# Retention and mixture of experts: fewer matmul sizes in the expert loop, one leaf above 336 rows, and the last empty scatters moved ahead

## What is computed

```
logits = x @ w_gate                      # 2304 x 8
expert = argmax(logits);  gate = softmax(logits)[expert]
h = maximum(x_of_expert @ w1[e], 0)      # 512 -> 1024
y = h @ w2[e]                            # 1024 -> 512
out[row] = gate[row] * y                 # at most 576 rows an expert are kept
```

## Time and profile before

| | us |
|---|---|
| median of 3 runs (lowest, highest) | 385.37 (383.69, 397.42) |
| the profiled execution | 389.81 |
| its span | 387.9 |
| TensorE matmul busy | 359.4 (93%) |
| VectorE, ScalarE, GpSimd busy | 218.2, 187.4, 136.1 |

### The profile page before, as it was taken

The page is one execution under the profiler, slowest core; times in us unless marked ns, Lnnn a source line. Parts: engine busy times, 40 slices in busy tenths (PEclk is TensorE's granted clock), DMA queues, the critical chain, the costliest instruction groups (busy, mean ns, idle before and its releaser), DMA issues.

```text
span 387.9 us, 10976 instructions
## 1 busy us (share of the span) xinstructions
PE 359.4 (93%) x3590; PEld 339.4 (88%) x3591; DVE 218.2 (56%) x450; ACT 187.4 (48%) x367; POOL 136.1 (35%) x131
## 2 busy tenths in 40 slices
PE   8999899999998899499979999999999999998980
PEld 4999799999875799499969999999999999998980
DVE  3136634938864585356545556656666756655740
ACT  1343433436330465256445547557657657646721
POOL 3655353533505222034404503532532432222205
PEclk9999999999995999789989999999999999999997
DMA  8889989887863599925533653664664654540001
GB/s 225 238 230 305 271 228 245 259 259 232 246 185 116 172 370 368 341 71 177 196 112 133 203 159 110 197 212 155 204 200 155 199 196 147 176 162 38 25 0 54
DMA packets 27435, 73.41 MB, mean 189 GB/s; under 512 B 7114, under 2 KB 7882, under 8 KB 27408
## 3 DMA queue, kind: packets, MB, share of 16 engines
q1 hardware_dynamic: 21008, 63.57, 51.9%
q0 software_dynamic: 6400, 9.46, 8.0%
HBM read 64.61 MB, written 19.92 MB: 218 GB/s over the span
## 4 chain that ended last, share of the span: by engine, by line
PE 86%; issue 4%; DVE 4%; DMA 3%; POOL 1%; ACT 1%; DVEq 0%; ACTq 0%; POOLq 0%; SPq 0%
PE bank L620 19%; PE bank L622 18%; PE bank L621 18%; PE bank L455 5%; PE bank L479 4%; PE bank L608 4%; PE bank L469 3%; PE bank L505 3%; PE bank L498 3%; PE bank L613 3%; PE bank L487 2%; DMA qk_raw<-in_qk 2%; PE bank L558 2%; DMA y_nat<-x_rows,slot_row 1%; POOL out L382 1%
## 5 line engine op out<-in xcount | busy, mean ns | idle before, releaser
L620 PE MATMUL bank<-m_hi,w_hi 128*128 x512 | 154.8, 302 | 3.0 <-DVE m_lo L1002 1.4
L621 PE MATMUL bank<-m_hi,w_lo 128*128 x512 | 152.9, 299 | 0.0
L622 PE MATMUL bank<-m_lo,w_hi 128*128 x512 | 152.8, 298 | 0.0
L827 DVE TENSOR_TENSOR w_lo<-w_raw,w_hi 128x512 fp32r<-128x512 f32 x128 | 88.5, 691 | 33.5 <-ACT w_hi L702 33.2
L620 PEld LDWEIGHTS bank<-m_hi,w_hi 128*128 128x128 f32 x512 | 96.3, 188 | 5.9 <-issue 5.8
L621 PEld LDWEIGHTS bank<-m_hi,w_lo 128*128 128x128 f32 x512 | 96.3, 188 | 0.0
L622 PEld LDWEIGHTS bank<-m_lo,w_hi 128*128 128x128 f32 x512 | 96.2, 188 | 0.0
L702 ACT ACTIVATE w_hi<-w_raw 128x512 fp32r<-128x512 f32 x128 | 79.9, 626 | 24.9 <-PE bank L622 24.9
L382 POOL DMA_INDIRECT out<-y_nat,slot_row x40 | 41.7, 1042 | 137.1 <-PE bank L622 88.9
L1006 DVE SCALAR_TENSOR_TENSOR m_lo<-bank,m_hi 128x384 fp32r<-128x384 f32 x64 | 35.7, 558 | 38.0 <-ACT m_hi L783 38.0
L376 POOL DMA_INDIRECT x_gat<-x_rows,slot_row x37 | 41.0, 1109 | 43.6 <-PE bank L622 22.6
(11 more groups left out here) (89 smaller groups left out, 369.6 us busy)
## 6 DMA issues: line engine op xcount, KB each, us to landing
w_raw<-in_moe_w SPq DMA_DIRECT2D x64, 512.0 KB, 3.8
qk_raw<-in_qk SPq DMA_DIRECT2D x24, 384.0 KB, 4.9
kv_raw<-in_kv SPq DMA_DIRECT2D x24, 384.0 KB, 5.9
x_rows<-x_nat SPq DMA_DIRECT2D x24, 192.0 KB, 5.2
out<-zeros SPq DMA_DIRECT2D x12, 384.0 KB, 7.7
q_dec<-in_qdecay SPq DMA_DIRECT2D x5, 192.0 KB, 6.2
out<-y_nat,slot_row POOLq DMA_INDIRECT x40, 2.8
x_gat<-x_rows,slot_row POOLq DMA_INDIRECT x37, 3.9
```

The source lines that it names most:

```text
L620: pe.matmul(dst, w_hi[:, s, i, :], hi[:, i, cols], start=(i == 0), stop=False)
L621: pe.matmul(dst, w_lo[:, s, i, :], hi[:, i, cols], start=False, stop=False)
L622: last = pe.matmul(dst, w_hi[:, s, i, :], lo[:, i, cols], start=False, stop=(i == K4 - 1))
L827: dve.tensor_tensor(w_lo[:, j % SLOTS], w_raw[j // 2][:, j % 2 * 512:j % 2 * 512 + 512].rearrange("p (k n) -> p k n", k=K4), w_hi[:, j % S ...
```

## The change

- `SIZES` is now 272, 288, 304, 320, 336. The leaves of 256 and of 384 columns are gone. Expert 7 (255 rows) runs 272 columns instead of 256; the other seven keep their size.
- All counts above 336 share one leaf, `large`, with 384 columns and a test of the count around each wide part. It stands ahead of the five small leaves in the program. None of the eight experts runs it.
- In `large` the wide product comes ahead of the narrow one.
- GpSimd issues the two wide scatters of expert 7 ahead of its three narrow ones. ScalarE counts up `b_y_scaled` of an expert without wide rows ahead of its products instead of behind them.
- `keep_warm` gets a parameter that nobody uses.

```diff
-SIZES = [256, 272, 288, 304, 320, 336, WA]
+SIZES = [272, 288, 304, 320, 336]
...
-def by_count(eng, count, body, sizes=(*SIZES, None)):
-
+def by_count(eng, count, body, large, sizes=None):
+
+    if sizes is None:
+        with eng.If(count > SIZES[-1]):
+            large()
+        with eng.Else():
+            by_count(eng, count, body, large, SIZES)
+        return
     if len(sizes) == 1:
-        body(*((WA, True) if sizes[0] is None else (sizes[0], False)))
+        body(sizes[0])
         return
     half = len(sizes) // 2
     with eng.If(count <= sizes[half - 1]):
-        by_count(eng, count, body, sizes[:half])
+        by_count(eng, count, body, large, sizes[:half])
     with eng.Else():
-        by_count(eng, count, body, sizes[half:])
+        by_count(eng, count, body, large, sizes[half:])
...
+            def wide_scatters(e):
+                for g in range(NA, NG):
+                    pool.wait_ge(b_y_scaled, NB * (e - 1) + g - NA + 1)
+                    after_chunk(e, g)
+                    scatter(e - 1, g)
+
             for e in range(E + 1):
...
+                if e == E:
+                    wide_scatters(e)
                 if e > 0:
                     for g in range(NA):
                         pool.wait_ge(y_scaled, NA * (e - 1) + g + 1 + SCALED0)
                         after_chunk(e, g)
                         scatter(e - 1, g)
-                    for g in range(NA, NG):
-                        pool.wait_ge(b_y_scaled, NB * (e - 1) + g - NA + 1)
-                        after_chunk(e, g)
-                        scatter(e - 1, g)
+                if e == E:
+                    break
+                if e > 0:
+                    wide_scatters(e)
...
-                        last = product(ring[s][:, 0:n], s, hi, lo, slice(0, n))
-                        if wide:
-                            last = product(wide_ring[s][:, 0:WB], s, hi, lo, slice(WA, CAP))
-                        last.then_inc(result_made, 1)
+                        if count is not None:
+                            with pe.If(count > WA):
+                                product(wide_ring[s][:, 0:WB], s, hi, lo, slice(WA, CAP))
+                        product(ring[s][:, 0:n], s, hi, lo, slice(0, n)).then_inc(result_made, 1)
...
+            def small(e, n):
+                pe.sem_inc(b_xs_tr, NB)
+                chunks(e, n)
+                pe.sem_inc(b_y_tr, NB)
+
+            def large(e, count):
+
+                with pe.If(count > WA):
...
+                        turn_x(wide_turn[g], NA + g).then_inc(b_xs_tr, 1)
+                with pe.Else():
                     pe.sem_inc(b_xs_tr, NB)
-                    chunks(e, n, False)
+                chunks(e, WA, count)
+                with pe.If(count > WA):
...
-                by_count(pe, count, lambda n, wide: sized(e, n, wide))
+                by_count(pe, count, lambda n: small(e, n), lambda: large(e, count))
...
                     act.sem_inc(b_xs_hi_made, NB)
+                    act.sem_inc(b_y_scaled, NB)
```

More of the change, by code:

```diff
@@ L553, in add_to_map, with keep_warm @@
                 return last
-            def keep_warm(times, unused=bank[6]):
+            def keep_warm(times, unused=bank[6], n=512):
                 for _ in range(times):
-                    pe.matmul(unused[0:C, :], zeros[:, 0:C], zeros[:, 0:512], start=True, stop=True,
+                    pe.matmul(unused[0:C, 0:n], zeros[:, 0:C], zeros[:, 0:n], start=True, stop=True,
                               skip_group_check=True)
@@ L623, in product, with chunks @@
                 return last
-            def chunks(e, n, wide):
+            def chunks(e, n, count=None):
                 with pe.Fori(0, CHUNKS // SLOTS) as it:
@@ L637, in chunks @@
                             pe.wait_ge(xs_lo_made, e * NA + NA)
-                        if s == 0 and wide:
+                        if s == 0 and count is not None:
                             pe.wait_ge(b_xs_lo_made, NB * (e + 1))
@@ L644, in chunks @@
                             pe.wait_ge(y_scaled, e * NA + SCALED0)
-                        last = product(ring[s][:, 0:n], s, hi, lo, slice(0, n))
-                        if wide:
-                            last = product(wide_ring[s][:, 0:WB], s, hi, lo, slice(WA, CAP))
-                        last.then_inc(result_made, 1)
-            def sized(e, n, wide):
-                if not wide:
-                    pe.sem_inc(b_xs_tr, NB)
-                    chunks(e, n, False)
-                    pe.sem_inc(b_y_tr, NB)
[L655 to L666, removed]
+                        if count is not None:
+                            with pe.If(count > WA):
+                                product(wide_ring[s][:, 0:WB], s, hi, lo, slice(WA, CAP))
@@ new lines, in chunks @@
+                        product(ring[s][:, 0:n], s, hi, lo, slice(0, n)).then_inc(result_made, 1)
[5 more added lines that the diff above has]
+                with pe.If(count > WA):
+                    pe.wait_ge(xs_lo_made, e * NA + 2 * NA)
+                    pe.wait_ge(y_scaled, e * NA + SCALED0)
+                    for g in range(NB):
+                        pe.wait_ge(gathered[NA + g], 16 * (e + 1))
+                        turn_x(wide_turn[g], NA + g).then_inc(b_xs_tr, 1)
+                with pe.Else():
+                    pe.sem_inc(b_xs_tr, NB)
+                chunks(e, WA, count)
+                with pe.If(count > WA):
+                    pe.wait_ge(result_copied, (e + 1) * CHUNKS + COPIED0)
+                    for g in range(NB):
+                        turn_y(wide_turn[g], NA + g, min(G, WB - g * G)).then_inc(b_y_tr, 1)
+                    pe.wait_ge(b_y_scaled, NB * (e + 1))
+                with pe.Else():
+                    pe.sem_inc(b_y_tr, NB)
@@ L805, in expert @@
                         scale_y(wide_turn[g], e + 1, NA + g, min(G, WB - g * G)).then_inc(b_y_scaled, 1)
-                else:
-                    act.sem_inc(b_y_scaled, NB)
             act.wait_ge(routed, 2)
```

## The result

The changed kernel takes 396.36 us (median of five runs, 392.47 to 397.53), beside 386.54 us (383.69 to 397.42, five runs) for the kernel before: 1.0253 times as long, interval 1.0207 to 1.0299. It is slower; the forecast was 380.0 us, range 371 to 389.5. The profiled execution took 396.61 us with a span of 394.6.

What follows compares the result with a forecast made beforehand. TensorE, busy 359.4 of 387.9 us, bounds the kernel, its loop idle mostly from two late exit branches. Terms -4.1 + 1.24 - 2.58 = -5.4 us, off the median of 385.37, gave 380.0 us, range 371 to 389.5.

Steps and rivals of the forecast that it cites:

- step 3: Entry of expert 0: the jump past the large leaf to the 272 leaf costs 0, at worst +5.4 us.
- The prediction's own sign of being wrong: An entry branch over 3 us, expert 0's first matmul at 134 us or later, or a short first exit.
- rival C: Expert 0's entry misses and both exits still do: 389.5 us, up to 395.8 with expert 1's entry; chance 0.12, upper end 0.05.
- 1. The exit of expert 0: Branch out of expert 0's leaf, over 540 instructions instead of 960: still a miss, taken as 0, at best -7.6 us.
- step 2: Branch out of expert 1's leaf, over 135 instructions instead of 550: no longer waits, -4.1 us.
- 4. Expert 7: Expert 7's matmuls: 272 columns instead of 256 cost +1.24 us, all on the path.
- 5. The tail: End of the kernel: two scatters fewer behind expert 7's first narrow one, -2.58 us.
- 6. The tests: Fourth compare ahead of the 320 and 336 leaves: at most +0.2 us in two passes, taken as 0.
- Rival D: Loop branches: the code's place changes nothing, both exits wait as they did; -1.3 us, 384.0 us; chance 0.10.

Runs made afterwards that it cites:

- e1: The changed kernel with the large leaf laid behind the five small ones, one If turned round; 382.74 us, 0.9833 of the kernel before.
- e5: The changed kernel without its leaf for more than 336 rows; 381.51 us, 0.9848 of the kernel before.
- e6: The changed kernel with a branch hint at the head of TensorE's loop for its jump to the small leaves; 384.22 us, 0.9965 of the kernel before.
- e7: The changed kernel with the large leaf behind the small ones, a second time; 382.24 us, 0.9869 of the kernel before.
- e3: The kernel before with 155 never-run matmuls between the head of the pass and the tests; 400.94 us, 1.0347 of the kernel before.
- e9: The kernel of small leaves alone (e5) with its five leaves reversed, 336 first and 272 last; 390.86 us, 0.9997 of the kernel before.
- e8: The changed kernel again, without an edit; median 392.99 us of six runs, its profiled execution 382.39 us.
- e2: The kernel before with only the change's scatters and count-up, TensorE's program untouched; 398.55 us, 1.0275 of the kernel before.
- e11: The kernel before, one more execution with its profile and no edit; 403.05 us.

## Why the prediction was wrong

The step that failed is **step 3**, the entry of expert 0. I took it as 0 "with little confidence" and gave +5.4 us as its bound. It cost +3.0 at the first matmul and +2.5 within expert 0, 5.5 us. In all three profiles of the changed kernel this branch waited (3843, 3799, 3324 ns), in e1, e5, e6 and e7, with the leaf last, without it or with a hint, it never did, and in e3 never-run code in its place brought it back. The prediction's own sign of being wrong, a first matmul at 134 us or later, came with 134.24. In the four profiles with never-run code in the way and no hint (the changed kernel's three, e3) this branch missed; in the others it missed only in e9, where the leaf itself stands far off. My ground was that TensorE stays in the block of the head for 16 us with the queue idle. That is so, and of no use: from 116.7 to 129.7 us no instruction packet came, and the branch at 128.7 us waited. Idle time did not bring in code past the block that is fetched ahead. The working for the first exit said so ("one fetched ahead"), and I did not hold the entry to the same rule.

The larger part is a term that the sum did not have, the **entry of expert 1**: +6.4 us up to its first matmul and +1.7 within it, 8.1 us. Only the far end of rival C named it, with +4.1. The jump over the large leaf had been made 38 us before, and waited again. For the entries I took code, once fetched, as kept; it is not always. The working had the sign: the loop's end, fetched behind expert 0, was missed again behind expert 1, and I wrote that such a target seems not to stay. I did not carry that to the entries. e8 against the first profile shows what this one place costs: 10.8 us between two executions of the same code, 6.33 against 15.27 us at the boundary.

What the entry wait of expert 0 is worth by itself can be told from e8, which has it but no miss at expert 1, and e7, which has neither. Their spans, 380.4 and 379.6 us, hide it, because e8 came to the tests earlier. The last transposes ahead of the tests, e8 and then e7:

```profile
124.81 1.55 PE L622 MATMUL bank<-ident,x_gat 128*128 128x128 f32 x12
```

```profile
127.77 1.47 PE L622 MATMUL bank<-ident,x_gat 128*128 128x128 f32 x12
```

From their end to the end of the span it is 254.1 us in e8, 250.4 in e7 and 250.9 in e1, the same code as e7. So the wait cost 3.1 to 3.7 us in these single executions: 5.1 us idle ahead of the first matmul instead of 0.4 to 0.6, and 1.9 us in expert 0, less 3.5 at the boundary behind it (6.33 for 9.82, e7). The time at which these transposes end lies between 124.6 and 132.6 us over all profiles, with no miss ahead of it, so the time of a first matmul alone says little about a branch.

The rest of the loss of the changed kernel is the entry of expert 1. By the times of its runs (10 of 12 in the long pattern, with both long profiles showing the two misses there) it nearly always has them, while the kernel before had long times in 16 of 43 runs. Both of its long executions with a profile, e2's (with its TensorE program) and e11, missed at the same five places.

The other steps:

1. The exit of expert 0 stays a miss: right (3741 ns). It was 2.0 us cheaper, which I had not foreseen. The last section says with what that goes together.
2. The exit of expert 1 is clean: right. 169 ns, and -3.6 us for -4.1. The boundary keeps 3.56 us, where one without a fourth test took 3.17.
4. Expert 7: +1.16 us for +1.24, right.
5. The tail: -2.9 us for -2.58, right. Two scatters at 1.29 us are 2.59 of it (5.16 - 2.57); e2 gives the same, -2.84.
6. The tests, taken as 0: 0.4 us over the five boundaries from expert 2 to expert 7, and 0.4 us in the one behind expert 1 (step 2).

So the sum should have read -2.0 + 5.5 + 8.1 - 3.6 + 1.2 - 2.9 + 0.4 = +6.7 instead of -5.4. Of the rivals, C had the sign, the place (entry of expert 0, then of expert 1) and, at its upper end of 395.8 us, the time. Its reason, that both exits still miss, was wrong for the second exit, and it had 0.05 of the chance. That its time came within 0.6 us was luck: it had the two entries at 5.4 + 2.2 + 4.1 = 11.7 us where they cost 13.6, and no gain at either exit where they gave back 5.6.

A second failing is that of the range. One of the three runs shown of the kernel before took 397.42 us, 12 us over the others. I read past it. e11 and e2 show what such a run is: more misses, at the entry of expert 1 and on to expert 3. A kernel with two times has to be forecast with both, and with what the change does to their shares.

Rival D rested on the rule in the Trainium skill, "Runtime: NRT & Kernel Launch", section "Instruction fetch mechanics", that a taken branch whose target is outside a window of two pages forces a fetch. For first visits the rows agree (3843 ns at the entry, 3741 ns at the exit). For later ones they do not: the L105 jump took 208 to 222 ns six times in a row, and no instruction packet of this queue came behind 182 us, in six more passes of a loop of some 1,060 instructions.

What stays open: why the code past the large leaf is there for expert 1 in some executions and gone in others. In the long executions the misses go on from expert 1, in the kernel before to expert 3, and in e1, e5, e6 and e7, where no entry jumped far without a hint, none of 28 runs was above 389 us. Which block is given up for which was not measured. That the first far jump starts the chain fits the changed kernel, but not e8, nor e2 and e11, where the entry of expert 0 did not wait (352 ns in e11).

The best version is e1's, run twice: the change as it is with the large leaf last, 382.74 and 382.24 us. It beats the kernel before (0.9833 and 0.9869, intervals above) and, on the same chip, the changed kernel (392.99). Four of the six runs of the latter are above all of e7's (378.44 to 384.76), the other two within them. All that the change does for time on its own (steps 2 and 5, less 4) is then left, and only the first exit waits.

## What to carry to other kernels

Code that never runs has a price if a branch must jump over it: lay out leaves so that the way from the tests to the leaf taken first is short, and put the rare large one last. Where the profile names "issue" ahead of the first instruction of a block, look at the sequencer's branches and at the instruction packets before at anything else, and count every far jump of the first two passes, entries as well as exits. Where a few runs of the same kernel lie 3% apart, take a profile of each kind before forecasting a change to it.

## What the runs showed of the hardware

**A hint moves a wait.** A prefetch hint made its own branch short each time (327, 332 and at most 476 ns), but with exit hints the next test waited 6177 and 5494 ns. Only the hint at the loop's head, ahead of a first far jump, paid (384.22 us for 392.99).

**How long a miss is goes with the other traffic.** The windows over the exit branch of expert 0, with the clock, DMA share and GB/s last: e8, e7, e5, e6.

```profile
156.52:159.98 3.46, 2.04 (x17) 1.82 (x15) 3.03 (x5) 1.40 (x3) 0.00 (x0) 1.00 0.74 265
```

```profile
152.78:157.81 5.03, 2.04 (x17) 1.82 (x15) 3.02 (x5) 1.40 (x3) 0.00 (x0) 0.96 0.92 323
```

```profile
156.49:162.45 5.96, 2.04 (x17) 1.82 (x15) 3.03 (x5) 1.40 (x3) 0.00 (x0) 1.00 1.02 393
```

```profile
151.05:158.55 7.50, 2.04 (x17) 1.82 (x15) 3.03 (x5) 1.40 (x3) 0.00 (x0) 0.80 1.00 381
```

In eleven profiles this branch missed. At a DMA share of 0.60 to 0.80 it took 3.5 to 3.7 us (the three of the changed kernel), at 0.91 to 1.02 it took 4.1 to 7.5 (the other eight). The four whose entry was late are these three and the one with 4.1, e3. I read from this that the weights, streaming in while TensorE stood still, were further ahead of it when expert 0 ended, and that the packet came sooner. This is how a wait of 3.8 us at the entry can have given 1.6 us (e8 for e7) to 2.2 us (3741 ns for 5903) back at the exit. In e8 the clock came with it: behind its exit it stays at 1.00, behind e7's it is at 0.50 for 6.8 us. In the first profile of the changed kernel it fell all the same. That the streams are the cause was not tried by taking them away.

**The wait is mostly for the packet to start.** Of the 36 misses in all profiles 35 ended 2.3 to 3.0 us after the last instruction packet that started during them (one 3.8), with the DMA engines idle or full. What differs is how late this packet starts: 0.9 to 1.2 us into the three short exit misses, 1.8 to 5.0 us into the eight long ones (5.0 in e6). The first miss at the entry of expert 1 has another reason to be long, for it took 5317 ns at a share of 0.03. Two packets came, where a miss at an exit of expert 0 has one. In the first profile of the changed kernel, from 166.2 to 169.2 us and from 169.2 to 172.0 us:

```profile
q8 instruction: 1, 0.02, 4.0%
...
q8 instruction: 1, 0.02, 2.2%
```

The first started 0.3 us ahead of the branch, the second 2.8 us into it, and the branch ended 2.5 us after that. In all seven profiles with a miss there an earlier packet stands ahead of the one that ends it in this way. The branch behaves as if it had to wait its turn behind a fetch already under way; what that packet holds the trace does not say.
